# Attention scores and read-outs of a chunked linear-attention kernel, moved from 128-row products with zero padding to four 64x64 array tiles

## The reference

```python
for t in range(S):
    kt, vt, rt = (k[:, :, t], v[:, :, t], r[:, :, t])
    wt, at, bt = (w[:, :, t], a[:, :, t], b[:, :, t])
    y[:, :, t] = np.einsum('bhd,bhde->bhe', rt, state)
    Sa = np.einsum('bhde,bhe->bhd', state, at)
    state_decay = state * wt[:, :, None, :] - np.einsum('bhd,bhe->bhde', Sa, bt)
    state = state_decay + np.einsum('bhd,bhe->bhde', vt, kt)
# then x = softmax-gated layer norm(x @ w_in) @ w_out, and (relu with slope)(x @ w_in2) @ w_out2
```

## Time and profile before

| what | value |
|---|---|
| median of 3 runs | 1035.43 us (1034.56 to 1040.74) |
| the profiled execution | 1041.0 us, span 1039.2 us |
| TensorE busy | 90% of the span |
| VectorE, ScalarE, GpSimd busy | 63%, 42%, 23% |
| mean granted TensorE clock | 0.959 |

### The profile page before, as it was taken

How to read it: one execution, slowest core, us unless ns; L and a number is a source line. 1 busy time by engine, 2 the same in 40 slices (tenths; PEclk the granted TensorE clock), 3 DMA queues, 4 the chain that set the end, 5 groups by cost and what they waited for, 6 DMA issues and landing times.

```text
span 1039.2 us, 32979 instructions
## 1 busy us (share of the span) xinstructions
PE 935.4 (90%) x14112; PEld 885.0 (85%) x14112; DVE 652.2 (63%) x1123; ACT 435.6 (42%) x890; POOL 234.4 (23%) x451
## 2 busy tenths in 40 slices
PE   2448989999998989748999999999999999999997
PEld 2347988898888878748999999999999999999987
DVE  8836867778787644565646556464746456564734
ACT  3314435444544522354534434353535345353522
POOL 7653555655666530000000000000000000000000
PEclk9659999999999998978999999999999999999999
DMA  5634555667566543053010000000000000000000
GB/s 146 122 87 104 132 123 127 146 156 178 120 137 148 123 90 99 23 165 94 1 26 1 27 1 26 20 6 25 0 25 0 25 0 25 5 21 13 1 14 13
DMA packets 143860, 67.44 MB, mean 65 GB/s; under 512 B 120012, under 2 KB 129356, under 8 KB 143740
## 3 DMA queue, kind: packets, MB, share of 16 engines
q1 hardware_dynamic: 141628, 65.53, 26.1%
q10 hardware_dynamic: 2112, 0.13, 0.1%
HBM read 45.98 MB, written 19.66 MB: 63 GB/s over the span
## 4 chain that ended last, share of the span: by engine, by line
PE 81%; DVE 10%; issue 4%; ACT 2%; DMA 1%; POOL 1%; ACTq 0%; SPq 0%; DVEq 0%; POOLq 0%
PE px L336 7%; PE acc L1018 6%; PE acc L1019 5%; PE acc L1020 5%; PE bank L1018 5%; PE bank L1020 5%; PE bank L1019 5%; PE mid L1018 4%; PE mid L1020 4%; PE mid L1019 4%; PE pq L393 4%; PE pr L360 2%; PE pr L349 2%; PE py L419 2%; PE pu L368 2%
## 5 line engine op out<-in xcount | busy, mean ns | idle before, releaser
L1247 POOL TENSOR_TENSOR stats<-stats 128x1 f32<-128x1 f32 x24 | 13.2, 549 | 583.7 <-DVE stats L1330 583.7
L1352 DVE SCALAR_TENSOR_TENSOR stage<-mid,w_raw 128x512 f32<-128x512 f32 x96 | 66.3, 691 | 110.2 <-ACT w_raw L1193 110.1
L1018 PE MATMUL acc<-wo_h,act_h 128*128 128x320 f32 x384 | 122.3, 319 | 6.5 <-DVE act_l L1261 6.5
L1189 ACT ACTIVATE stage<-mid 128x512 f32<-128x512 f32 x96 | 57.3, 597 | 162.3 <-PE mid L1072 162.3
L1019 PE MATMUL acc<-wo_h,act_l 128*128 128x320 f32 x384 | 119.2, 311 | 0.0
L1020 PE MATMUL acc<-wo_l,act_h 128*128 128x320 f32 x384 | 119.2, 311 | 0.0
L1018 PE MATMUL mid<-zT_h,w_h 128*128 128x256 f32 x384 | 108.6, 283 | 0.7 <-DVE zT_s L1261 0.7
L1020 PE MATMUL mid<-zT_l,w_h 128*128 128x256 f32 x384 | 108.6, 283 | 0.0
L1019 PE MATMUL mid<-zT_h,w_l 128*128 128x256 f32 x384 | 108.6, 283 | 0.0
L761 POOL TENSOR_TENSOR al<-al,prod 40x512 f32<-40x512 f32 x48 | 70.2, 1463 | 118.4 <-DMA al<-a_features_first 80.5
L1193 ACT ACTIVATE w_raw<-stage,minus_alpha 128x256 f32<-128x256 f32 x192 | 87.3, 502 | 3.1
(11 more groups left out here) (152 smaller groups left out, 2400.8 us busy)
## 6 DMA issues: line engine op xcount, KB each, us to landing
wkb<-wkb_features_first SPq DMA_DIRECT2D x46, 242.5 KB
rvu<-rv_features_first SPq DMA_DIRECT2D x48, 160.0 KB
l_scr<-lb SPq DMA_DIRECT2D x24, 256.0 KB, 4.3
x_scr<-x SPq DMA_DIRECT2D x24, 256.0 KB, 3.7
al<-a_features_first SPq DMA_DIRECT2D x48, 80.0 KB
sv<-v_time_first SPq DMA_DIRECT2D x48, 80.0 KB, 4.7
out<-y_sb SPq DMA_DIRECT2D x12, 320.0 KB, 2.3
d_scr<-s_x SPq DMA_DIRECT2D x12, 256.0 KB, 2.4
```

Of the source, the lines that this page charges most:

```text
L1018: pe.matmul(o, left[0], right[0], start=start, stop=False)
L1189: act.activation(neg[q % 2][:], mid[q % 2][:], ACT.Relu, scale=-1.0).then_inc(neg_ready, 1)
L1352: dve.scalar_tensor_tensor(out=act_f[q % 2][:], in0=mid[q % 2][:], scalar=0.0, in1=slope[q % 2][:], op0=ALU.max, op1=ALU.add).then_inc(act ...
```

## The change

Scores and read-outs are computed for each head as four products of 64 rows by 64 columns, one for each batch element (`half`, which picks the rows of the array) and slot (which picks its columns). Each batch element writes to a bank of its own, where the two shared a bank side by side. `a_bd`, its memset, its semaphores and `spread_a` go; the scores read `al` as it is. Semaphores count once where they counted two pieces; `copy_l` and `mask_ka` handle all 8 heads of one batch element at once. In TensorE's step, `state` moves from behind `turn_state` to just behind `outputs`, VectorE's `next_state` moves ahead of `mask_q`, and ScalarE's `spread_state` ahead of `take_state`. `mask_ka` moves behind the second `take_horner` as a whole.

```diff
+    QUADS = [(0, 0), (1, 1), (0, 1), (1, 0)]
...
-        def scores(m, piece):
-            pe.wait_ge(kbT_ready, m + 1)
-            pe.wait_ge(a_bd_ready, 2 * m + 2)
...
-            for i in range(4):
-                h = piece * 4 + i
-                for slot in range(2):
-                    ins = pe.matmul(banks[HR[slot], h * P:(h + 1) * P], kbT[m % 3][:, h, slot], a_bd[:, :, h],
-                                    start=True, stop=True)
-            ins.then_inc(l_done, 1)
+        def scores(m, part):
+            if part == 0:
+                pe.wait_ge(kbT_ready, m + 1)
+                pe.wait_ge(a_ready, 2 * m + 2)
...
+            for h in range(part * 4, part * 4 + 4):
+                for half, slot in QUADS:
+                    col = half * 512 + h * T
+                    ins = pe.matmul(banks[HR[slot], col:col + T], kbT[m % 3][ER[half], h, slot],
+                                    al[m % 7][ER[half], half, h], start=True, stop=True)
+            if part == 1:
+                ins.then_inc(l_done, 1)
...
-            for piece in range(2):
-                wait(pe, q_ready, 2 * m - 1 + piece)
-                for h in range(piece * 4, piece * 4 + 4):
-                    for slot in range(2):
-                        ins = pe.matmul(pq[HR[slot], h * P:(h + 1) * P], vuT[m % 3][:, slot, h], r_bd[m % 3][:, :, h],
-                                        start=True, stop=True)
-                ins.then_inc(q_done, 1)
+            wait(pe, q_ready, 2 * m)
+            for h in range(NH):
+                for half, slot in QUADS:
+                    col = half * 512 + h * T
+                    ins = pe.matmul(pq[HR[slot], col:col + T], vuT[m % 3][ER[half], slot, h],
+                                    r_bd[m % 3][ER[half], half, h], start=True, stop=True)
+            ins.then_inc(q_done, 1)
...
-                dve.tensor_tensor(al[m % 7][other, half, piece * 4:piece * 4 + 4], src[other, :, half],
-                                  repeated(later, other, 4), ALU.mult).then_inc(ka_ready, 1)
+            src = heads(score_banks(m)[:, half * 512:half * 512 + 512], NH, T)
+            dve.tensor_tensor(al[m % 7][other, half], src[other], repeated(later, other, NH), ALU.mult)\
+               .then_inc(ka_ready, 1)
...
-        def spread_a(m):
-
-            if m == 0:
-                act.wait_ge(a_bd_set, 1)
-            act.wait_ge(a_ready, 2 * m + 2)
-            wait(act, l_done, 2 * m)
-            for half in range(2):
-                act.copy(a_bd[ER[half], half], al[m % 7][ER[half], half]).then_inc(a_bd_ready, 1)
-
```

More of the change, by code:

```diff
@@ L289, in tensor @@
     def tensor(pe):
-        def scores(m, piece):
-            pe.wait_ge(kbT_ready, m + 1)
-            pe.wait_ge(a_bd_ready, 2 * m + 2)
[L294 to L299, removed]
-            banks = score_banks(m)
-            for i in range(4):
-                h = piece * 4 + i
-                for slot in range(2):
-                    ins = pe.matmul(banks[HR[slot], h * P:(h + 1) * P], kbT[m % 3][:, h, slot], a_bd[:, :, h],
-                                    start=True, stop=True)
-            ins.then_inc(l_done, 1)
+        def scores(m, part):
+            if part == 0:
+                pe.wait_ge(kbT_ready, m + 1)
+                pe.wait_ge(a_ready, 2 * m + 2)
+                if m < AHEAD:
+                    before = m - 2 if m < AHEAD - 1 else m - 1
+                    wait(pe, l_ready, 2 * before + 2)
+                    wait(pe, ka_ready, 2 * before + 2)
+                else:
+                    pe.wait_ge(kbn_ready, 2 * m)
+            banks = score_banks(m)
+            for h in range(part * 4, part * 4 + 4):
[5 more added lines that the diff above has]
+                ins.then_inc(l_done, 1)
         def turn_kb(m):
@@ L442, in step @@
                 outputs(n - 1)
+            if n + 2 < NG:
+                state(n)
             read_out(n)
@@ L488, in scale_kb, with mask_ka, mask_q @@
                               ALU.mult).then_inc(kbT_ready, 1)
[L490 to L494, removed]
-            for half in range(2):
[L496 to L500, removed]
-                dve.tensor_tensor(al[m % 7][other, half, piece * 4:piece * 4 + 4], src[other, :, half],
-                                  repeated(later, other, 4), ALU.mult).then_inc(ka_ready, 1)
[L504 to L510, removed]
+        def mask_ka(m, half):
+            if half == 0:
+                dve.wait_ge(l_done, m + 1)
+                wait(dve, rhs_done, m - 6)
+            other = HR[1 - half]
+            src = heads(score_banks(m)[:, half * 512:half * 512 + 512], NH, T)
+            dve.tensor_tensor(al[m % 7][other, half], src[other], repeated(later, other, NH), ALU.mult)\
+               .then_inc(ka_ready, 1)
+        def mask_q(m, half):
+            if half == 0:
+                dve.wait_ge(q_done, m + 1)
+                wait(dve, y_done, m)
+            dve.tensor_tensor(q[:, :, half], heads(pq[:, half * 512:half * 512 + 512], NH, T),
+                              repeated(later, slice(0, P), NH), ALU.mult).then_inc(q_ready, 1)
         def next_state(m):
@@ L614, in step @@
                 store_y(n - 1)
+            if n + 2 < NG:
+                next_state(n)
             mask_q(n, 0)
@@ L629, in step @@
             if front:
-                mask_ka(n + AHEAD, 1)
+                mask_both(n + AHEAD)
             if nxt:
@@ L645, in scalar, with copy_l @@
     def scalar(act, beside):
-        def copy_l(m, piece):
-            act.wait_ge(l_done, 2 * m + 1 + piece)
+        def copy_l(m):
+            act.wait_ge(l_done, m + 1)
             wait(act, x_done, 4 * (m - 6) + 1)
-            src = score_banks(m)[:, piece * 512:piece * 512 + 512].rearrange("p (n a t) -> p n a t", n=4, a=2)
             for half in range(2):
                 own = HR[half]
-                if m >= AHEAD:
-                    wait(act, ka_ready, half * (4 * m + 2 * piece + 1))
-                act.copy(lb[m // 2 % 3][own, m % 2, piece * 4:piece * 4 + 4], src[own, :, half]).then_inc(l_ready, 1)
+                src = heads(score_banks(m)[:, half * 512:half * 512 + 512], NH, T)
+                act.copy(lb[m // 2 % 3][own, m % 2], src[own]).then_inc(l_ready, 1)
         def take_rhs(m):
```

49 lines of the change are left out of this document (14 added, 35 removed).

## The result

The changed kernel takes 1065.21 us (median of four, 1061.09 to 1075.75) against 1035.80 us: 1.0252 times the kernel before, 95% interval 1.0204 to 1.0300, +29.4 us where +13 was forecast. The profiled execution took 1061.09 us, 20.1 more than that of before. Run again beside other kernels, the change gave 1.0281 and 1.0291.

A forecast was written before the change was run, and what follows sets the result against it. TensorE, 90% busy, was taken as the engine to count, with instruction fetch setting the changed step's pace. +15.5 us for 18 steps, -1.5 for last steps, -1 for prologue: +13 on 1035.4 gives 1048.5 us, range 1016 to 1066.

The forecast's parts named there:

- Hidden fetch: Rival, 22%: instruction fetch stays hidden, so steady steps keep a 1.3 us gain each; 1010 us, up to 1025.
- the four tiles don't take turns: Denies a rival: column tiles alternate, so read-outs and scores gain nothing; 1027 us if fetch is hidden, no separate chance.
- part (4): Steady step: 992 instructions for 864, 3.875 blocks of 256 for 3.375; the fetch sets the pace at 16.3 us.
- 18 x (16.3 - 15.44) = 15.5 us: Loss over the 18 of 24 steps that have scores, each going from 15.44 to 16.3 us.
- 3.875 x 4.2 = 16.3 us: Steady step's length: 3.875 instruction blocks times an assumed mean fetch round of 4.2 us.
- Part (1): Read-outs and scores as 64x64 tiles: 0.93 us each for 1.76, saving 1.6 us of TensorE per step.
- Part (2): Tiling changes per step fall from nine to five at 0.12 us each: -0.5 us.
- Part (3): Other engines: VectorE masks -0.3 us; waits for `hh` ahead of horner 2 and 3; 13.5 us a step if instructions are there.
- The small terms: Outside the main sum: last steps 1.5 us less under lighter DMA traffic, prologue 1 us less without memset and `a_bd` wait.
- The signs it named: Changed profile, 100 to 347 us: "issue" 40 us or more, mostly between read-out and horner 3; q8 packets about 4.2 us apart.

The follow-up runs named there:

- split: Kernel before, each score and read-out product of 128 columns issued as two of 64, without the new tiles and order; 1.0215 times the kernel before.
- rows64: Changed kernel with its tiles fed 64 rows in place of 40, the other 24 holding zeros; 1.0176 times the kernel before.
- wide_tiles: Changed kernel with 128 moving columns in each score and read-out tile, the 64 surplus ones written over; 1.0245 times the kernel before.
- after_again: The changed kernel unaltered, run once more on the same chip as its comparison kernels; 1.0281 times the kernel before.
- wide_steady: Changed kernel with 128 moving columns per tile only in the 18 steps with both read-out and scores; 1055.94 us, 1.0179 times the kernel before.
- after_third: The changed kernel unaltered, run on one chip beside the kernel wide only in steady steps; 1069.21 us, 1.0291 times the kernel before.
- quads_old_order: Changed kernel with `state` and `next_state` in their old places; 1063.79 us for the profiled execution, no ratio given.
- quads_bf16: Changed kernel reading the upper 16 bits of score and read-out operands as bf16, 864 instructions a step for 992; 0.9926 times the kernel before.
- early_quads: Kernel before with the new state order, and the four tiles for the scores of the first six groups alone; 1037.16 us, 0.9939 times the kernel before.
- light_before: Kernel before with most data DMAs of the attention cut to a few elements from the third group on, output wrong; 0.9838 times the kernel before.

## Why the prediction came out as it did

**Direction and mechanism: right.** More instructions cost more than the tiles give; split shows it without the tiles and the order. "Hidden fetch", which the Trainium skill's page "Runtime: NRT & Kernel Launch" (Instruction fetch mechanics) would have, is refuted here by 29.1 us of "issue", and the four tiles don't take turns: 64 records in 0.98 us.

**What failed: the last step of part (4), "so the fetch sets the pace", which gave 16.3 us for a step.** Measured are 16.90, 16.90 and 17.10 us in three profiles of the changed kernel, so the term 18 x (16.3 - 15.44) = 15.5 us should have been 26 to 30 us. That reasoning multiplied a mean round by all 3.875 blocks and took TensorE's own work, 12.3 us at full clock, as hidden behind it. The runs show two things in its place.

First, the own work is 14.8 us: 13.0 us where the clock is full, and 1.8 us more because the clock stands at 1.2 GHz for 4.7 us of each step. The sum had no term for the clock.

Second, own work isn't hidden. TensorE stands for instructions 30 times in 62 blocks; in the others its own pace counts, and as only one block is held ahead, by the prediction's reading, a block that TensorE uses up slowly isn't paid back by a quick one. The prediction itself had said so of `outputs` and had not applied it to the right side, which takes 7.0 us at half clock for 3.9. Part of the 1.8 us falls in time that would have been a stop. What doesn't is seen in pairs of kernels with the same instructions: 0.5 us a step in rows64 against the changed kernel, 0.6 in wide_tiles against after_again and in wide_steady against after_third. These are net gains, rows64 with only 41 of 75 us at 1.2 GHz gone, the two others after paying for 1.5 us more of array work, so the price of the clock is at least 18 x 0.5 to 0.6 = 9 to 11 us; the direct test of it, wide_steady, gives 12 to 13 us in the whole kernel, 10.2 us of them in the 16 steps by the profiles.

**How much of 3.875 x 4.2 = 16.3 us was right.** The rounds between stops are 4.35 us in the mean, near the 4.2 that was chosen, and the kernels with 992 instructions and a clock of 0.96 or more take 16.32, 16.46 and 16.58 us. But this is in part luck: these have 14.5 to 15 us of own work at full clock, where 12.3 was forecast, and the changed kernel's steps at full clock, with 13.0 us, are far shorter: 14.40 and 14.62 us in the two that are shown. Whether the clock is full there because the stops are short, or the other way round, isn't shown.

**Part (1), the tiles:** 0.93 us forecast for the read-out, 0.98 measured, the switch at its end included. The scores are slower. One half of the heads in a step at full clock, up to the next horner stage:

```profile
136.46 0.27 PE L305 MATMUL pa<-al,wkb 40*64 40x64 f32 x2
...
136.52 0.66 PE L305 MATMUL pa<-al,wkb 40*64 40x64 f32 x30
137.17 0.69 PE L338 MATMUL px<-hh,lower 64*32 64x32 f32 x32
```

These are 0.7 us, so 1.4 us in a step where 0.93 was forecast. That is most of what the own work of 13.0 us lies above 12.3; why they are slower than the read-out in the same tiles is open.

**Part (2), switches:** no run removes them alone. quads_old_order has two more than the changed kernel, and its step isn't longer (16.85 for 16.90 us), so 0.2 us isn't visible beside the rest. **Part (3):** `hh` was to be waited for 1.2 us in a step if instructions are there. In quads_bf16 it is 18.0 us in 15.5 steps, 1.2 us (with shorter products, which leave less cover); in the changed kernel only 2.8 us in all, since the stops for instructions stand in the same place.

**The small terms** went both ways. The three profiles of the changed kernel (after, after_again, after_third) beside that of before, cut at the marks:

| stretch | forecast | measured |
|---|---|---|
| up to the third step | -1 us | -4.5, -6.8, -5.2 us |
| the 16 steps | 16 x 0.86 = +13.8 us | +23.2, +23.3, +26.5 us |
| from there to the end | 2 x 0.86 - 1.5 = +0.2 us | +0.1, +4.6, +5.0 us |

In the prologue the wait for `a_bd` was worth more than 1 us (early_quads, which has the tiles there alone, begins its third step 3.6 us early). The last steps gained nothing from the lighter traffic, with stops and a granted clock from 347 to 440 us of 0.89 for 0.93. In the whole kernel, +13 us was forecast, wide_steady shows +15.3 (medians) to +18.6 us (ratio) without most of the half clock, and after_third +28.6 us.

**The signs it named.** "Issue" grew to 29.1 us, not to 40 or more: at half clock, TensorE's work fills part of the stops (rows64, with less of it, has 34.9 us). Most of it does lie between read-out and horner 3. Packets are 247 / 56 = 4.4 us apart, not 4.2.

What stays open: why the clock falls. The length of the stops doesn't decide it: split has 19.3 us of them and 128 rows at work (0.99), quads_bf16 has 18.8 us and 40 rows with shorter products (0.83), though that one also waits 18.0 us for `hh`. light_before has the old tiles and nearly no stops (1.00), the changed kernel stops and 64 by 64 tiles fed 40 rows (0.86), and 64 rows or 128 moving columns in those tiles lift it to 0.93 and 0.99. So what the array is given matters. A run with 64 by 64 tiles and no stops wasn't made, so whether stops are needed at all is not shown.

## What to carry to other kernels

A smaller tile of the array is paid in instructions: count the instructions of a step in blocks of 256, and hold the round of the fetch, as the trace shows it, against TensorE's own time block by block before counting any gain of the array: a dense block stops, and a slow one adds its own time without paying the stop back. Where the result makes TensorE stop with a lighter load, ask for a second price, the granted clock, and look for it in the durations of lines that the edit doesn't touch. A kernel that costs the array more work in the right places only (wide_steady) tells the clock from the fetch, where the total of a cruder one (wide_tiles) hides it; and an edit that loses in the steady loop can still start it earlier (early_quads, by its trace).

## What the runs showed of the hardware

Four fp32 tiles of 64 by 64 do run side by side: 64 records in 0.98 us, for 1.88 us of 32 records of 128 columns. Where TensorE uses a block of 256 instructions up before the next is there, it goes on 4.1 us after it last went on even where data DMAs use only 0.26 of the engines, so some 60 instructions per us is what a long dense stretch got here. And a kernel that moved 128 columns where 64 were wanted was 1.1% faster in all, with the granted clock at 0.96 in place of 0.86; 64 rows for 40, at the same instructions, lifted it from 0.86 to 0.93.
